# New order of the loads of a fused kernel's front, and 28 identity turns in place of 36

## The chip, the cores and the metric

The kernel runs on one core of a Trainium2 chip. Its engines are TensorE (PE, matrix products), VectorE (DVE), ScalarE (ACT), GpSimd (POOL) and SyncE (SP), which issues DMA transfers. Time is the device time of one execution in microseconds (us); the figure of a kernel is the median of its runs.

## The reference

A small two-way attention between 512 tokens and 32 states per head, for 8 batches and 8 heads, is followed by a gated layer and by a second layer with a tanh. Cut to what is computed:

```python
scores = scale * np.matmul(x, state.transpose(0, 1, 3, 2))      # tokens read the states
a = softmax(scores);  xread = np.matmul(a, state)
scores2 = scale * np.matmul(state, x.transpose(0, 1, 3, 2))     # states read the tokens
a2 = softmax(scores2); sread = np.matmul(a2, x)
x = rows of np.concatenate([xread, sread], axis=2)              # 8 * 544 rows of 512
h = (x @ w1) * (x @ w2) @ w3                                    # w1, w2: 512 x 1024, w3: 1024 x 1024
x = h @ w_out                                                   # 1024 x 512
h = x @ w_in;  return (h - np.tanh(h)) @ w_out2                 # 512 x 2048, 2048 x 512
```

All data are float32. A product is made of three passes over two parts of each operand, a high part (fp32r, written by ScalarE) and a low part (the rest, written by VectorE).

## The kernel before, in words

The stages run one after the other on every engine: the front (`stage_front`), the states' rows (`stage_ys`), the first layer (`stage_moe1`) and the second (`stage_moe2`). Only the front is touched, some 80 us at the start.

The front does three things beside each other. It multiplies w3 by w_out once and for all, in 8 rounds of 4 pieces: round r takes a block of 512 KB of w3 (`load_w3`, L390), split by ScalarE into w3T_hi (L440, L446) and by VectorE into w3T_lo (L563, L568), times the 8 parts k of w_out (`load_wo`, L378; wos_hi L450, wos_lo L573), of which a piece takes two; the matmuls are at L724, and the last of a round raises `prod_done`. It does the states' attention for 8 batches e: `scores` (L682, from xT, the columns of x, 1024 KB a batch, and raising `scored`) into the PSUM room px, ScalarE's copy (L473) and exp (`exp_a2`, L481), PE's turn of it (L690), `sread` (L702, from xs, the rows of x, 1024 KB a batch, raising `sread_done`) and a turn of its result (`sread_turn`, L710), from which ScalarE and VectorE make srs_hi (L500) and srs_lo (L603). And it loads w1 and w2 in 8 parts of 512 KB (`load_w`, L385: four quarters of the rows, w1 and w2 in turn) into a room of their own, w_raw, with no wait ahead. ScalarE's `split_w(0)` (L469) waits for all 8, and VectorE's follows it (L581); these are needed first by `s1` (L752), at the front's end.

PE's order is written out by hand: `warm()` (L670) turns the identity WARM times into px, with no use of the result; then pieces 0 to 4, scores(0), pieces 5 to 7, scores(1), a2_turn(0), and for each further batch e the pieces up to `PIECES_AT[e]`, sread(e - 1), scores(e + 1), sread_turn(e - 2) and a2_turn(e). `scores(e)` also waits until the exp of batch e - 1 has emptied px (L677). At the end come piece 31, sread_turn(6), sread(7), the first value products (L112) and s1.

The orders of ScalarE and VectorE are written out too. ScalarE's, around the first batches, is: empty_prod(0), copy_st(0), split_w3(2), exp_a2(0), empty_prod(1), copy_st(1), turn_a2(0), exp_a2(1), split_w3(3). After the last batch's exp it is split_w(0), split_w(1), copy_sr(6), split_sr(5) and so on, and VectorE's is the same with L603 for split_sr.

SP issues nearly all loads, in its own order, on one queue. Three kinds wait first, because their two buffers are used in turn: xT of batch e for `scored` of batch e - 2, xs of batch e for `sread_done` of batch e - 2, and w3 of round r for `prod_done` of round r - 2. A wait holds up all that stands behind it in SP's order. xT and xs of batches 0 and 1 wait for nothing. ScalarE issues the first w_out load and the first two loads of the states.

Of the kernel before, what the change touches and what calls it, by code (L numbers as in the profile page):

```python
# [51 lines left out]
def after(eng, sem, count):  # L52

    if not (isinstance(count, int) and count <= 0):
        eng.wait_ge(sem, count)
# [14 lines left out]

PASSES = ((0, 0), (0, 1), (1, 0))
LAST = len(PASSES) - 1
WARM = 36
WRING = 3


# [219 lines left out]
def stage_front(nc, sem, room_a, room_b, room_c, room_o, small, w_at, x_rows, x_cols, state_cols, w1, w2, w3_cols, wo, aT, w34_at, w34,  # L296
# [71 lines left out]
    def load_xT(eng, e):  # L368

        after(eng, scored, e - 1)  # L370
        eng.dma_start(xTb[e % 2][:, :, :], x_cols[e]).then_inc(xT_in[e % 2], 16)

    def load_xs(eng, e):

        after(eng, sread_done, e - 1)
        eng.dma_start(xsb[e % 2][:, :, :], x_rows[e]).then_inc(xs_in[e % 2], 16)

    def load_wo(eng, n):  # L378
        ks = slice(WO_LOADS[n][0], WO_LOADS[n][-1] + 1)
        eng.dma_start(wor[:, ks, :], wo.rearrange("(k p) c -> p k c", p=P)[:, ks, :]).then_inc(wo_in[n], 16)  # L380

    def load_sT(eng, n):
        eng.dma_start(sT[:, STATES[n], :, :], state_cols[:, STATES[n], :, :]).then_inc(sT_in[n], 16)

    def load_w(eng, n):  # L385

        q, ab = n // 2, n % 2
        eng.dma_start(w_raw[:, q, ab, :], (w1, w2)[ab][q * P:(q + 1) * P, :]).then_inc(w_in[ab], 16)

    def load_w3(eng, r):  # L390

        after(eng, prod_done, r - 1)
        eng.dma_start(w3r[r % 2][:, :, :], w3_cols[r]).then_inc(w3_in[r % 2], 16)

    def sync(sp):
        def load_first(n):
            sp.dma_start(w3r[0][:, FIRST[n], :], w3_cols[0, :, FIRST[n], :]).then_inc(first_in[n], 16)

        for n in range(2):
            load_first(n)  # L400
        for n in range(1, len(WO_LOADS)):
            load_wo(sp, n)
        load_w3(sp, 1)
        load_xT(sp, 0)
        load_w3(sp, 2)
        load_xT(sp, 1)
        load_xs(sp, 0)
        load_sT(sp, 2)
        load_xT(sp, 2)
        load_w3(sp, 3)  # L410
        load_xs(sp, 1)
        load_xT(sp, 3)
        load_w3(sp, 4)
        load_w(sp, 0)
        for e in range(2, 5):
            load_xs(sp, e)
            load_xT(sp, e + 2)
            load_w(sp, e - 1)
            if e < 4:
                load_w3(sp, e + 3)  # L420
        load_xs(sp, 5)
        load_xT(sp, 7)
        load_w3(sp, 7)
        for n in (4, 5):
            load_w(sp, n)
        load_xs(sp, 6)
        for n in (6, 7):
            load_w(sp, n)
        load_xs(sp, 7)

    def gpsimd(pool):
        pool.memset(ident[:, :], 0.0).then_inc(ident_zeroed, 1)  # L432
# [232 lines left out]
    def tensor(pe):  # L665
        def warm():

            pe.wait_ge(ident_ready, 1)
            for n in range(WARM):
                pe.transpose(px[:, 0:P], ident[:, :], ident[:, :])  # L670
# [109 lines left out]
        for f in range(NF1):  # L780
            s1(f)

    return {"sync": sync, "gpsimd": gpsimd, "scalar": scalar, "vector": vector, "tensor": tensor,
            "signals": (pst, s1_done, s1_pm, s1_lo)}

# [695 lines left out]
```

## Time and profile before

| | us |
|---|---|
| median of 3 runs | 1248.16 |
| lowest and highest | 1247.09, 1248.64 |
| the profiled execution, its time | 1246.85 |
| its span, first to last instruction | 1245.1 |
| PE busy | 1237.0 |
| VectorE busy, ScalarE busy | 800.1, 548.5 |
| mean granted clock of PE | 1.000 |

The page gives the busy time of each engine as a share of the span. The share says which engine could be the bound; where it is not quite 100%, the list of waits says who made it stand. Times of the timeline count from the span's start. In it, a number in brackets is the idle time of the engine ahead of the instruction, and after the arrow stands what ended it. A matmul's end is modelled, and the next one begins before it, so the distance of two starts is the pace. "To landing" of a load is counted from the start of its issue on SP to the moment when its semaphore is raised.

### The profile page before, as it was taken

The page shows a single profiled execution, that of the slowest core. Times are in us where ns is not written, and L with a number is a line of the kernel's source. Part 1 is how long each engine was busy: PE and PEld are TensorE (multiplying, and loading weights), DVE is VectorE, ACT ScalarE, POOL GpSimd, SP SyncE. Part 2 cuts the span into 40 slices and gives each one's busy share as a digit, 9 for nine tenths or more (in the row PEclk, how much of TensorE's full clock was granted, in tenths as well). Part 3 has the DMA queues.
Part 4 walks back from the last instruction along what each step waited for, and adds up shares of the span by engine and source line. Part 5 has one row for each costly group of instructions (what it writes and reads, how often), then busy time and mean ns, then how long its engine had stood idle before and what let it go on. Part 6 is the DMA issues. An engine that isn't in the chain of part 4 may idle for free.

```text
span 1245.1 us, 17116 instructions
## 1 busy us (share of the span) xinstructions
PE 1237.0 (99%) x6636; PEld 1004.5 (81%) x6636; DVE 800.1 (64%) x1295; ACT 548.5 (44%) x1028; POOL 1.3 (0%) x7
## 2 busy tenths in 40 slices
PE   9999999999999999999999999999999999999998
PEld 7779777777777778888888888888888888888887
DVE  4656556555555445878676676676676776766776
ACT  6663434333333334555444444444444444444444
POOL 0000000000000000000000000000000000000000
PEclk9999999999999999999999999999999999999999
DMA  9941000000000111311101001001001001010000
GB/s 354 372 172 52 35 34 1 34 35 1 34 35 1 68 71 49 93 60 34 51 18 40 12 18 52 1 18 51 0 17 51 8 8 51 17 42 0 9 34 18
DMA packets 17630, 63.76 MB, mean 51 GB/s; under 512 B 1968, under 2 KB 3376, under 8 KB 12960
## 3 DMA queue, kind: packets, MB, share of 16 engines
q1 hardware_dynamic: 16832, 62.00, 13.6%
q8 instruction: 40, 0.66, 0.2%
q10 hardware_dynamic: 704, 0.85, 0.2%
q14 instruction: 22, 0.18, 0.0%
q0 software_dynamic: 32, 0.07, 0.0%
HBM read 45.09 MB, written 17.83 MB: 51 GB/s over the span
## 4 chain that ended last, share of the span: by engine, by line
issue 100%; POOLq 0%; POOL 0%
POOLq L261 0%; POOL ident L434 0%; POOL ident L432 0%; POOLq L434 0%; POOLq L1469 0%
## 5 line engine op out<-in xcount | busy, mean ns | idle before, releaser
L1256 ACT ACTIVATE hq<-bank 128x512 f32<-128x512 f32 (+1 forms) x144 | 82.8, 575 | 393.8 <-PE bank L1382 393.8
L1327 DVE TENSOR_TENSOR hw<-hw,hq 128x512 f32<-128x512 f32 (+1 forms) x144 | 95.5, 663 | 193.5 <-ACT hw L1267 193.4
L1382 PE MATMUL bank<-ysp_hi,wi_hi 128*128 128x512 f32 (+1 forms) x576 | 217.4, 377 | 0.0
L1382 PE MATMUL bank<-ysp_lo,wi_hi 128*128 128x512 f32 (+1 forms) x576 | 217.2, 377 | 0.0
L1382 PE MATMUL bank<-ysp_hi,wi_lo 128*128 128x512 f32 (+1 forms) x576 | 217.2, 377 | 0.0
L1409 PE MATMUL wide<-wz_hi,gsp_hi 128*128 128x512 f32 x544 | 212.3, 390 | 0.3 <-DVE gsp_lo L1317 0.3
L1409 PE MATMUL wide<-wz_lo,gsp_hi 128*128 128x512 f32 x544 | 211.8, 389 | 0.0
L1409 PE MATMUL wide<-wz_hi,gsp_lo 128*128 128x512 f32 x544 | 211.7, 389 | 0.0
L1382 PEld LDWEIGHTS bank<-ysp_hi,wi_hi 128*128 128x128 f32 x576 | 108.2, 188 | 21.3 <-DVE gb L1346 0.9
L1382 PEld LDWEIGHTS bank<-ysp_lo,wi_hi 128*128 128x128 f32 x576 | 108.3, 188 | 20.6
L1382 PEld LDWEIGHTS bank<-ysp_hi,wi_lo 128*128 128x128 f32 x576 | 108.3, 188 | 19.9
L1409 PEld LDWEIGHTS wide<-wz_hi,gsp_hi 128*128 128x128 f32 x544 | 102.2, 188 | 22.2 <-DVE gsp_lo L1317 1.4
L1409 PEld LDWEIGHTS wide<-wz_hi,gsp_lo 128*128 128x128 f32 x544 | 102.1, 188 | 21.4
L1409 PEld LDWEIGHTS wide<-wz_lo,gsp_hi 128*128 128x128 f32 x544 | 102.1, 188 | 20.4
L1317 DVE TENSOR_TENSOR gsp_lo<-gb,gsp_hi 128x512 fp32r<-128x512 f32 (+1 forms) x144 | 95.5, 663 | 13.4 <-ACT gsp_hi L1249 0.5
L1071 PE MATMUL wide<-psp_hi,w_hi 128*128 128x512 f32 x256 | 101.5, 396 | 0.1
L1344 DVE COPY_PREDICATED gb<-far,wide 128x512 f32<-128x512 uint8 (+1 forms) x144 | 100.9, 701 | 0.2
L1071 PE MATMUL wide<-psp_lo,w_hi 128*128 128x512 f32 x256 | 99.8, 390 | 0.0
L1071 PE MATMUL wide<-psp_hi,w_lo 128*128 128x512 f32 x256 | 99.6, 389 | 0.0
L1346 DVE TENSOR_TENSOR gb<-bank,gb 128x512 f32<-128x512 f32 (+1 forms) x144 | 95.3, 662 | 5.0
L1334 DVE SCALAR_TENSOR_TENSOR gb<-hw,bank 128x512 f32<-128x512 f32 (+1 forms) x144 | 93.8, 651 | 0.1
L1249 ACT ACTIVATE gsp_hi<-gb 128x512 fp32r<-128x512 f32 (+1 forms) x144 | 86.2, 599 | 3.5 <-DVE gb L1346 3.3
(122 smaller groups left out, 1740.7 us busy)
## 6 DMA issues: line engine op xcount, KB each, us to landing
xT<-in_x_cols SPq DMA_DIRECT2D x8, 1024.0 KB, 10.2
xs<-in_x_rows SPq DMA_DIRECT2D x8, 1024.0 KB, 9.6
y_dram<-ysb SPq DMA_DIRECT2D x8, 1024.0 KB, 3.9
out<-ysb SPq DMA_DIRECT2D x8, 1024.0 KB, 4.6
yr<-y_dram SPq DMA_DIRECT2D x28, 256.0 KB, 4.0
w_raw<-in_moe_w SPq DMA_DIRECT2D x8, 512.0 KB, 11.2
wi_raw<-in_moe_w_in SPq DMA_DIRECT2D x4, 1024.0 KB, 6.5
raw<-in_moe_w_out SPq DMA_DIRECT2D x16, 256.0 KB, 2.6
```

The lines of the kernel that those rows point to most:

```text
L1071: mm = pe.matmul(py[c], w34[s][:, f, c * P:(c + 1) * P], psp[t][:, f % 2, :], start=f + m == 0, stop=f == NF1 - 1 and m == LAST)
L1249: act.activation(gsp[0][:, slot, 0:w], gb[:, slot % 2, 0:w], ACT.Copy).then_inc(g_hi, 1)
L1256: act.activation(hq[:, f % 2, 0:w], ph[f % 2][:, 0:w], ACT.Square).then_inc(sq_done, 1)
L1317: dve.tensor_tensor(gsp[1][:, slot, 0:w], g, plain(gsp[0][:, slot, 0:w]), ALU.subtract).then_inc(g_lo, 1)
L1327: dve.tensor_tensor(u, u, q, ALU.mult).then_inc(w2_done, 1)
L1334: dve.scalar_tensor_tensor(g, u, 1.0, h, ALU.add, ALU.mult).then_inc(near_done, 1)
L1344: dve.copy_predicated(g, far[:, f % 2, 0:w], pq[f % 2][:, 0:w]).then_inc(sel_done, 1)
L1346: dve.tensor_tensor(g, h, g, ALU.subtract).then_inc(g_done, 1)
L1382: mm = pe.matmul(ph[f % 2][:, 0:w], wi[s][c][:, f * P:(f + 1) * P], ysp[k][u][c][:, 0:w], start=c + m == 0, stop=c == KC - 1 and m == LAST)
L1409: mm = pe.matmul(po[j], gsp[s][:, f % 4, j * P:(j + 1) * P], wz[u][:, f, :], start=f + m == 0, stop=f == NF2 - 1 and m == LAST)
```

## The change

SP's order of the front's loads is rewritten. xT of batch 1 goes ahead of w3 of round 2. The halves of w1 and w2 come earlier: two ahead of w3 of round 4, two ahead of round 5, one each ahead of rounds 6 and 7 and the last two behind xT of batch 7. xs of batch 5 goes ahead of w3 of round 7 and xT of batch 7 behind it, and xs of batch 6 behind the last halves. The waits that each load carries stay as they are, and so do the number of loads and their sizes. WARM falls from 36 to 28.

```diff
-WARM = 36
+WARM = 28
@@ sync of stage_front
         load_w3(sp, 1)
-        load_xT(sp, 0)
+        for e in range(2):
+            load_xT(sp, e)
         load_w3(sp, 2)
-        load_xT(sp, 1)
         load_xs(sp, 0)
         load_sT(sp, 2)
         load_xT(sp, 2)
         load_w3(sp, 3)
         load_xs(sp, 1)
         load_xT(sp, 3)
+        for n in (0, 1):
+            load_w(sp, n)
         load_w3(sp, 4)
-        load_w(sp, 0)
-        for e in range(2, 5):
-            load_xs(sp, e)
-            load_xT(sp, e + 2)
-            load_w(sp, e - 1)
-            if e < 4:
-                load_w3(sp, e + 3)
+        load_xs(sp, 2)
+        load_xT(sp, 4)
+        for n in (2, 3):
+            load_w(sp, n)
+        load_w3(sp, 5)
+        load_xs(sp, 3)
+        load_xT(sp, 5)
+        load_w(sp, 4)
+        load_w3(sp, 6)
+        load_xs(sp, 4)
+        load_xT(sp, 6)
+        load_w(sp, 5)
         load_xs(sp, 5)
+        load_w3(sp, 7)
         load_xT(sp, 7)
-        load_w3(sp, 7)
-        for n in (4, 5):
-            load_w(sp, n)
-        load_xs(sp, 6)
         for n in (6, 7):
             load_w(sp, n)
-        load_xs(sp, 7)
+        for e in (6, 7):
+            load_xs(sp, e)
```

## Rows read from the trace of the kernel before

**Rows 1.** The page, busy time, share and instructions of each engine.

```profile
PE 1237.0 (99%) x6636; PEld 1004.5 (81%) x6636; DVE 800.1 (64%) x1295; ACT 548.5 (44%) x1028; POOL 1.3 (0%) x7
```

**Rows 2.** Waits of PE, whole run: waited for, us in total, times, longest.

```profile
PE wide L670 <- POOL ident L434: 1.5, 1, 1.5
PE wide L710 <- DVE srs_lo L603: 1.4, 1, 1.4
PE bank L724 <- DVE w3T_lo L568: 0.4, 1, 0.4
...
PE wide L682 <- DMA xT<-in_x_cols: 0.3, 1, 0.3
```

**Rows 3.** Timeline of SP: start us, us, engine, line, operation.

```profile
4.82 0.44 SPq L371 DMA_DIRECT2D xT<-in_x_cols  x1
13.73 0.33 SPq L393 DMA_DIRECT2D w3r<-in_w_cols  x1
...
20.80 0.43 SPq L376 DMA_DIRECT2D xs<-in_x_rows  x1
21.59 0.33 SPq L371 DMA_DIRECT2D xT<-in_x_cols  x1
```

**Rows 4.** DMA issues, the same four in turn: KB each, us to landing.

```profile
xT<-in_x_cols SPq DMA_DIRECT2D x1, 1024.0 KB, 9.5
...
w3r<-in_w_cols SPq DMA_DIRECT2D x1, 512.0 KB, 3.9
...
xs<-in_x_rows SPq DMA_DIRECT2D x1, 1024.0 KB, 10.0
...
xT<-in_x_cols SPq DMA_DIRECT2D x1, 1024.0 KB, 11.7
```

**Rows 5.** Windows of 1 us: busy per engine, PE clock, DMA share, GB/s.

```profile
14.00:15.00 1.00, 1.00 (x7) 0.57 (x5) 0.63 (x1) 0.34 (x1) 0.00 (x0) 1.00 0.29 49
...
40.00:41.00 1.00, 1.00 (x6) 0.81 (x6) 0.97 (x4) 0.65 (x2) 0.00 (x0) 1.00 0.37 115
```

**Rows 6.** Timeline of ScalarE: w_out, w3 of round 2, exp_a2(0), split_w(0).

```profile
7.85 3.33 ACT L450 ACTIVATE wos_hi<-wor 128x512 fp32r<-128x512 f32 x6 [0.90 <-DMA wor<-in_moe_w_out]
...
17.66 1.06 ACT L446 ACTIVATE w3T_hi<-w3r 128x1024 fp32r<-128x1024 f32 x1 [0.45 <-DMA w3r<-in_w_cols]
...
19.95 0.20 ACT L481 ACTIVATION_READ_ACCUMULATOR a<-wide,tbias 128x1 f32 x1
...
74.85 2.01 ACT L469 ACTIVATE w_hi<-w_raw 128x1024 fp32r<-128x1024 f32 x2 [1.60 <-DMA w_raw<-in_moe_w]
```

**Rows 7.** Timeline of VectorE: the later six wos_lo, and srs_lo before 78.9.

```profile
8.52 3.70 DVE L573 TENSOR_TENSOR wos_lo<-wor,wos_hi 128x512 fp32r<-128x512 f32 x6 [0.58 <-ACT wos_hi L450]
...
78.50 0.27 DVE L603 TENSOR_TENSOR srs_lo<-wide,srs_hi 128x128 fp32r<-128x128 f32 x1
```

**Rows 8.** Timeline of PE: first product, scores(0), scores(1), and from 78.9.

```profile
7.49 0.48 PE L724 MATMUL bank<-wos_hi,w3T_hi 128*128 128x512 f32 x1
...
9.35 0.47 PE L724 MATMUL bank<-wos_hi,w3T_hi 128*128 128x512 f32 x1 [0.23 <-DVE wos_lo L573]
...
14.67 0.39 PE L724 MATMUL bank<-wos_hi,w3T_lo 128*128 128x512 f32 x1
14.99 1.09 PE L682 MATMUL wide<-xT,sT 64*32 64x512 f32 x16
...
20.01 0.39 PE L724 MATMUL bank<-wos_hi,w3T_lo 128*128 128x512 f32 x1
20.41 1.09 PE L682 MATMUL wide<-xT,sT 64*32 64x512 f32 x16
...
78.91 0.30 PE L710 MATMUL wide<-ident,sr 128*128 128x128 f32 x1 [1.39 <-DVE srs_lo L603]
79.14 1.10 PE L702 MATMUL wide<-xs,a2T 128*32 128x64 f32 x64
```

**Rows 9.** Timeline of PE, the identity turns: to 5.3 us, and after 5.7 us.

```profile
1.53 4.10 PE L670 MATMUL wide<-ident 128*128 128x128 f32 x18 [1.53 <-POOL ident L434]
...
5.43 2.19 PE L670 MATMUL wide<-ident 128*128 128x128 f32 x17
```

## The prediction

> **What bounds the kernel now.** I read the shares by engine first [rows 1]: TensorE (PE) is busy in 1237.0 of a 1245.1 us span, so the change can win only idle time of PE, and only in the front, since no other line of code is touched. Then the waits of PE over the whole run [rows 2]. They are few: 1.5 us for the identity at the very start, 1.4 us at L710 for VectorE's srs_lo, 0.4 at L724 for w3T_lo, 0.3 at L682 for an xT load, 0.2 at L724 for wos_lo. The rest of the 8.1 us lies after the front or behind PE's last instruction. Everything past about 82 us goes PE's pace, so what the front gives or costs reaches the end of the run unchanged.
>
> Third, what stands behind these waits. They are transfers. The one queue of SyncE (SP) lands its loads in the order of issue, and with a backlog the landings stand 2.5 us apart per 1024 KB: the load issued at 20.80 lands at 30.8, the next, issued at 21.59, at 33.3 [rows 3, 4]. Half a megabyte takes 1.25. But the DMA engines are not always fed: their share drops to 0.29 between 14 and 15 us, because SP, having issued xT of batch 0 at 4.82, waits until 13.73 for prod_done before w3 of round 2, and xT of batch 1 stands behind that wait [rows 3, 5]. There is another hole at 40 us (0.37), and a slack stretch from 49 to 53 us. What is lost there is missing at the end: the last w lands at 74.7; ScalarE, free since 73.25, has sat 1.60 us for it and starts split_w(0) at 74.85; and the chain split_w, split_w, VectorE's L603 (78.50 to 78.77) lets PE go on at 78.91 [rows 6 to 8].
>
> **Part 1, the order of loads.** I redo the queue with those paces: a load lands 2.5 us per MB after the one ahead of it, but not sooner than a load issued to an empty queue, which is 3.9 us for 512 KB (w3 of round 2 [rows 4]). The sT load in small packets and the xT behind it keep the 4.4 us that they take together now. A time "before" is the start of the issue plus its time to landing; of some 30 such pairs four stand in [rows 3, 4].
>
> Issued early, xT of batch 0 lands at 14.3 as before (4.82 + 9.5) and xT of batch 1, now right behind it, at 16.8 in place of 20.1. Then w3 round 2 at 18.05 (before 17.6), xs0 20.6, xT2 24.9 (before 27.0), w3 round 3 26.2, xT3 31.2, w of w1 and w2 33.7, w3 round 4 34.9 (before 34.5), xT4 39.9, two more halves of w1 and w2 42.4. These halves are what sits in the queue when SP gets past prod_done for round 5 at 39.8: it lands at 43.9 (before 44.1) and the hole at 40 us is gone. xs3 46.5, xT5 49, w 50.3. At 48.4 w3 round 6 meets a queue as shallow as before, so I take most of that loss over: 52.7 (before 53.0), xs4 between 54.8 (at pace) and 57.1 (as before), taken 56.3 since the nearest rows are the old ones. From there a backlog holds: xT6 58.8 (before 59.7), xs5 62.5, w3 round 7 63.8 (before 67.2), xT7 66.3 (before 66.0), the last w 68.8 (before 74.7), xs6 71.3 (before 72.2), xs7 73.9 (before 77.2).
>
> Now PE's stalls. (a) 0.3 us (0.27 in PE's timeline) for xT6 at 59.7 goes [rows 2]: it lands 0.9 us earlier. (b) 0.4 us (0.38) at 69.6 for w3T_lo of round 7 goes: the load is 3.4 us earlier, and ScalarE, which now sits 1.7 us for it, splits it that much sooner. (c) 1.39 us at 78.9: with the last w in by 68.8, ScalarE starts split_w(0) when it is free, at 73.25 and not 74.85 [rows 6]. From that start to the end of L603 it takes 78.77 - 74.85 = 3.9 us, so L603 ends at 77.2. PE's idle time of 1.39 before 78.91 starts at 77.5 [rows 8], so PE could go on there. It fits with some 0.2 us to spare: PE's order, not VectorE, is late next. Sum: 2.04 us won.
>
> (d) A new wait is made. w3 round 2 now stands behind a megabyte more: 18.05 in place of 17.6. ScalarE waits for it already (L446 at 17.66, idle 0.45 before), and behind L446 in its order stands exp_a2(0), whose last piece ends at 20.15 [rows 6]. scores(1) on PE reuses px and waits for that exp (L677); it starts at 20.41, 0.40 after the last matmul's start, where scores(0) took 0.32 (14.67 to 14.99), so no slack is left there [rows 8]. I charge the full 0.45 us. Bounds: 0, if the fuller queue moves w3 sooner than the sum says, and 0.55. Other loads that land later than now (w3 round 4 by 0.4, xT7 by 0.3 at most 1.1) have over 1 us and, xT7, 0.7 us before PE needs them at 67.01, and 0.2 to 0.4 us at worst would show. The SP issues themselves are as many as before, 0.33 to 0.44 us each, and no wait is added; xT7 and xs5 change sides of the wait for prod_done of round 7, but the queue has over 5 us of backlog then.
>
> Part 1: -2.04 + 0.45 = -1.6 us.
>
> **Part 2, 28 turns for 36.** The first 18 start 0.217 us apart (1.53 to 5.22), the later ones 0.12 (the 17 from 5.43 end at 7.62, the last of 0.27 us) [rows 9]. This is TensorE's clock going from 1.2 to 2.4 GHz at some 5.5 us, after 4 us of work, though the granted clock reads 1.00 throughout. Eight late turns are 8 x 0.12 = 0.96 us, so the product could start at 6.53 and not 7.49. It can: the first wos_lo is there at 6.4, on a row of VectorE's that is not shown. But after two k (1.4 us) PE needs the third wos_lo, made from a wor load for which ScalarE waits until 7.85, the first of the six that VectorE writes from 8.52 on, 0.62 us each; PE starts on it at 9.35 now and will start on it at 9.35 then [rows 6 to 8]. So in this execution the 0.96 us only turn the gap of 0.23 into one of about 1.2 us: worth 0.
>
> In other executions it may be worth something. If the clock rises later than at 5.5 us, each turn costs 0.217: 36 of them at that step end at 9.3, 28 end at 7.6. The product would then reach the third k at up to 10.8 with 36 turns and still about in time with 28. So part 2 is worth 0 to 1.4 us; the only row I have says 0, and the median of before is 1.3 us above the profiled execution, so I take 0.3.
> The Trainium skill (TensorE: Matmul & The Clock Gate, Part 1: The HAM clock gate) says that the half rate is the default, that sustained activity releases it, and that the point where it is released differs from run to run. The trace agrees on the two rates; no run here shows yet whether the point moves. By that page fewer turns with a longer gap behind them speak against this change; the third rival below is what that would do here.
>
> **The sum.** Against the profiled execution (span 1245.1, time 1246.85): 1246.85 - 1.6 = 1245.3, without part 2. The median of the three runs is 1248.16; with part 2: 1248.16 - 1.6 - 0.3 = 1246.3 us.
>
> **Rivals.**
> 1. The new wait does not come, or part 2 is worth its upper part: -2.04 and -0.3 to -1.0, 1245.4 us. For it: DMA engines that finish early pass on to the next load, and the sum goes by the slowest. Against: ScalarE waits for exactly this load today. 0.22.
> 2. The 1.4 us stall is only renamed: PE waits at L710, or for xs7 at the next step, because the margin at 77.5 is 0.2 us and xs4 to xs6 come late. Then only (a) and (b) count: -0.65 + 0.45 = -0.2, 1247.9 us. Against: ScalarE is idle 1.60 us there, and every input but w is in place. 0.12.
> 3. Slower: the clock falls back in the gap of 1.2 us near 8 to 9.3 us. Price: at the start PE ran 4.0 us at half rate; a second such stretch costs half of it, 2.0 us, and pushes everything behind it, w3 round 2 too. -1.6 + 2.0 = +0.4, 1248.6 us, and more if the low level lasts on; it decides from the moment when two such stretches occur, or one costs over 1.6 us. Against: PE idled 1.39 us at 77.5 and came back at full pace (64 matmuls of L702 in 1.10 us, as everywhere) [rows 8]. 0.06.
> 4. The change does nothing to the time: the holes refill elsewhere (49 us, behind the new w halves) and the last w lands late all the same. 1248.1 us. It would take over 4 us of new loss, and the holes of today together cost 6. 0.04.
>
> **How the numbers follow.** Forecast 0.56, rivals 0.22, 0.12, 0.06, 0.04. 0.2% is 2.5 us, about the least that a measurement can tell from no change. The forecast, 1.9 us, lies inside, and so do rivals 2 and 4; rival 1 (2.8 us) is mostly beyond. With the scatter of the median runs (1247.09 to 1248.64) I give faster 0.24, same 0.73, slower 0.03. The range runs from 1244.9 (rival 1 with most of part 2) to 1248.2 (rival 2 and the scatter).
>
> **What would show it.** In the profile after: no stall at L682 near 59, at L724 near 69 and at L710 near 77; ScalarE's L469 starts right behind the last L481, near 73; DMA share near 1 from 13 to 16 us; the last w in by 69; L446 of round 2 at about 18.1 and scores(1) at about 20.85; L724 starts at 6.5 and has its gap of 1.2 us up to 9.35; weight loads of 0.19 us right after it. Wrong would be: matmuls of L724 over 0.3 us apart after 9.35 (rival 3), scores(1) still at 20.41 (rival 1), or L710 waiting for srs_lo or L702 for xs (rival 2).

## The result, and the profile after

The changed kernel takes 1252.16 us (median of 10 runs, 1250.26 to 1254.21) against 1247.74 for before (10 runs): ratio 1.0036, interval 1.0027 to 1.0046. It is slower by 4.4 us where a gain of 1.9 was forecast. The profiled execution took 1250.26 us, its span is 1248.5, 3.4 more than before's.

The page of the changed kernel, shares and instruction packets, and the same queue's row of before, 40 packets:

```profile
PE 1236.2 (99%) x6628; PEld 1002.8 (80%) x6628; DVE 800.8 (64%) x1295; ACT 548.5 (44%) x1028; POOL 1.3 (0%) x7
...
q8 instruction: 58, 0.95, 0.3%
```

```profile
q8 instruction: 40, 0.66, 0.2%
```

TensorE is busy as long as before [rows 1], so the loss is idle time. PE's waits in the changed kernel, which answer to [rows 2] (its lines are numbered 5 higher: L675 for L670, L729 for L724, L1387 for L1382):

```profile
PE bank L1387 <- issue: 4.2, 2, 2.1
PE wide L675 <- POOL ident L439: 1.5, 1, 1.5
PE bank L729 <- DVE wos_lo L578: 1.5, 2, 1.3
PE wide L687 <- ACT a L486: 0.8, 1, 0.8
```

The three stalls of the front that the change aimed at are gone (L715 for srs_lo, L729 for w3T_lo, L687 for xT). In their place stand a wait at L687 for ScalarE's exp, 0.8 us, and, first in the list, two waits of 2.1 us at L1387, in the second layer, with no releaser at all. Nothing of the diff is there.

The front gained what it should. The next rows are from the timelines: SP, where the states' rows are stored, first in the kernel before and then in the changed one; and of the changed kernel ScalarE's split of w3 round 2 and split_w(0), and PE:

```profile
118.75 0.66 SPq L794 DMA_DIRECT2D y_dram<-ysb  x1
```

```profile
117.18 0.66 SPq L799 DMA_DIRECT2D y_dram<-ysb  x1
```

```profile
18.65 1.06 ACT L451 ACTIVATE w3T_hi<-w3r 128x1024 fp32r<-128x1024 f32 x1 [1.34 <-DMA w3r<-in_w_cols]
...
73.31 2.00 ACT L474 ACTIVATE w_hi<-w_raw 128x1024 fp32r<-128x1024 f32 x2
```

```profile
9.47 0.47 PE L729 MATMUL bank<-wos_hi,w3T_hi 128*128 128x512 f32 x1 [1.32 <-DVE wos_lo L578]
...
21.30 1.09 PE L687 MATMUL wide<-xT,sT 64*32 64x512 f32 x16 [0.80 <-ACT a L486]
...
77.36 0.30 PE L715 MATMUL wide<-ident,sr 128*128 128x128 f32 x1
```

ScalarE splits w at 73.31 with no idle time ahead, where [rows 6] had 74.85; PE is at L715 at 77.36, not 78.91 [rows 8]. At 117 us the changed kernel leads by 118.75 - 117.18 = 1.57 us. By the end it is 3.4 behind: 5.0 us are lost after that, in two places. The first one, PE's timeline:

```profile
839.49 0.49 PE L1387 MATMUL bank<-ysp_hi,wi_hi 128*128 128x512 f32 x1
839.82 0.40 PE L1387 MATMUL bank<-ysp_lo,wi_hi 128*128 128x512 f32 x1
842.28 0.50 PE L1387 MATMUL bank<-ysp_hi,wi_lo 128*128 128x512 f32 x1 [2.07 <-issue]
```

The second is its twin at 1018.78. L1387 there is the first step of `tile(2 * i, 0)`, inside the only loop that TensorE runs as a loop, `with pe.Fori(1, PAIRS)` in `stage_moe2`: three rounds, so two jumps back. After each jump PE gets two matmuls done and stands; from start to start it is 842.28 - 839.82 = 2.46 us where 0.23 is usual. Around the jump the DMA engines carry nothing but code. The changed kernel between 836 and 846 us; the first line is the DMA engines' share in 40 slices of 0.25 us, and its three digits stand for packets at 836.8, 839.9 and 844.1:

```profile
DMA  0002000000000002000000000000000020000000
DMA packets 3, 0.05 MB, mean 5 GB/s; under 512 B 0, under 2 KB 0, under 8 KB 0
q8 instruction: 3, 0.05, 1.9%
```

In the same ten microseconds of the kernel before no packet moves at all. From 845 to 1200 us the changed kernel fetches 15 such packets, and before none. 0.95 MB in 58 packets is 16 KB each.

The trace also holds TensorE's branch instruction itself (the timeline above leaves such instructions out). At its two jumps back it takes 3.40 and 3.29 us in the changed kernel, begun at 835.81 and 1012.41, and 0.24 and 0.22 us in the kernel before. During the branch PE still works off matmuls that were handed to it earlier, up to the one at 839.24, so that wait does not show. What shows is the next one: the branch ends at 839.2, two matmuls follow, a packet moves at 839.9, and PE goes on at 842.28.

**Theory A, the layout of the code.** A turn is a weight load and a matmul; PE's count falls by 8 of each. So the loop's code lies 16 instructions earlier, and by this theory its start has slipped over the edge of a fetched block. The loop then touches one block more than TensorE keeps, so each jump back has to wait for code. **Rivals.** B: the new order of loads does it, by when the transfers meet the loop. C: fewer turns are bad as such, through the clock at the start, or in proportion to their number.

### The profile page after: what moved, and what is told of

It reads as the page before. It is cut to its first block, busy times and chain, and to the rows that moved or that the text cites. A ratio compares the mean times of both kernels' runs of the same rounds, so it can differ in the third digit from the quotient of the medians.

```text
span 1248.5 us, 17100 instructions
## 1 busy us (share of the span) xinstructions
PE 1236.2 (99%) x6628; PEld 1002.8 (80%) x6628; DVE 800.8 (64%) x1295; ACT 548.5 (44%) x1028; POOL 1.3 (0%) x7
## 4 chain that ended last, share of the span: by engine, by line
issue 100%; POOLq 0%; POOL 0%
POOLq L261 0%; POOL ident L439 0%; POOL ident L437 0%; POOLq L439 0%; POOLq L1474 0%
## 5 line engine op out<-in xcount | busy, mean ns | idle before, releaser
L1387 PE MATMUL bank<-ysp_hi,wi_lo 128*128 128x512 f32 (+1 forms) x576 | 217.5, 378 | 4.2 <-issue 4.2
L1387 PE MATMUL bank<-ysp_hi,wi_hi 128*128 128x512 f32 (+1 forms) x576 | 217.6, 378 | 0.0
L1387 PE MATMUL bank<-ysp_lo,wi_hi 128*128 128x512 f32 (+1 forms) x576 | 217.3, 377 | 0.0
L1387 PEld LDWEIGHTS bank<-ysp_hi,wi_lo 128*128 128x128 f32 x576 | 108.3, 188 | 24.9 <-issue 5.0
L1387 PEld LDWEIGHTS bank<-ysp_hi,wi_hi 128*128 128x128 f32 x576 | 108.2, 188 | 21.7 <-DVE gb L1351 1.0
L1387 PEld LDWEIGHTS bank<-ysp_lo,wi_hi 128*128 128x128 f32 x576 | 108.3, 188 | 20.4
```

Source lines behind the costliest of these rows:

```text
L1387: mm = pe.matmul(ph[f % 2][:, 0:w], wi[s][c][:, f * P:(f + 1) * P], ysp[k][u][c][:, 0:w], start=c + m == 0, stop=c == KC - 1 and m == LAST)
```

## The experiments

All are compared with runs of before on the same chip, in the same job. Medians of before in the three jobs: 1247.47, 1247.29 and 1247.48 us.

**One part at a time.** The first has the order of before and 28 turns.

```diff
-WARM = 36
+WARM = 28
```

> The order of loads of before, and 28 turns in place of 36. Theory A (code layout): 8 turns fewer are 16 instructions fewer on TensorE ahead of the loop of the second layer, and the loop then starts at the end of a fetched block of code; at each of its two jumps back TensorE stands about 2.1 us for code. Expected: two idle times of about 2.1 us at L1382 by no named releaser, about 58 instruction packets in place of 40, span 1245.1 + 5.0 = 1250, median 5 to 6.5 us above before. Theory B (the new order of loads does it, by shifting when transfers meet the loop): no such idle times here, time as before within 1 us. Theory C (the clock falls after the gap near 8 us): the matmuls of L724 behind 9.4 us stand over 0.3 us apart.

Measured 1253.43 us, ratio 1.0052 (1.0038 to 1.0066): the turns alone cost 6 us. Its page has 58 instruction packets, and among its first waits of PE are

```profile
PE bank L1382 <- issue: 4.6, 2, 2.4
...
PE wide L710 <- DVE srs_lo L603: 1.4, 1, 1.4
```

Theory B falls: the order of loads is that of before, and so is the stall at L710. The second takes the new order and puts the turns back.

```diff
-WARM = 28
+WARM = 36
```

> The new order of loads, and 36 turns. Theory A: TensorE's code has the length of before, so 40 instruction packets, no idle time at L1387, and what the order is worth in the front remains: 1.2 to 1.6 us below before (the stalls of 0.3, 0.4 and 1.4 us gone, a new one of 0.8 us at scores(1)). Theory B: 3.4 us or more above before, with the two idle times.

Measured 1245.82 us, ratio 0.9985 (0.9976 to 0.9994), 40 packets, no wait at L1387. The order alone gains 1.65 us between medians, as the prediction's part 1 had it.

**The same 28 turns at the start, with the length of the code restored.** The 8 turns come back where PE stands idle anyway.

```diff
         warm()
-        pieces(0, 5)
+        pieces(0, 1)
+        for n in range(8):
+            pe.transpose(px[:, 0:P], ident[:, :], ident[:, :])
+        pieces(1, 5)
```

> The new order of loads, 28 turns at the start and the other 8 behind the first piece of the product, where TensorE stands idle for 1.3 us. Theory A: the code ahead of the loop is as long as before, so 40 instruction packets, no idle time at L1387, 1.2 to 1.8 us below before. If it were the 28 turns as work ahead of the first product (the clock, theory C) or the order (B): as the changed kernel, 3.4 us or more above before.

Measured 1245.88 us, ratio 0.9989 (0.9980 to 0.9998), 40 packets, no wait at L1387. This is against C in its plain form: TensorE has as few turns before its first product as in the changed kernel, and nothing is lost. But the 8 turns also fill the gap behind the first product, so this run doesn't say what the gap does. The run with no jump, further down, does: it keeps 28 turns and a gap of 1.30 us, and loses nothing.

**Where the edge is.** The new order with 32, 31 and 30 turns, a step of two instructions for each turn.

```diff
-WARM = 28
+WARM = 32
```

> The new order of loads and 32 turns: 8 instructions fewer than before, 8 more than the changed kernel. In the changed kernel TensorE gets through two matmuls (4 instructions) of the repeated loop before it stands. Theory A: with 8 instructions more ahead, the loop's start lies behind the edge of the block, so no idle time at L1387, 40 packets, 1.2 to 1.8 us below before. A cause that grows with the number of turns taken away would give half of the loss: about 1 to 2 us above before.

> The new order and 31 turns, between 30 (stands for code before the first matmul of each repetition) and 32 (does not). One turn is 2 instructions. All or nothing again: 40 packets and about 2 us below before, or 58 packets and about 5 us above. I expect no stall, since with 30 turns not even one matmul came ahead of it.

> The new order and 30 turns: 4 instructions more than the changed kernel, which gets through 4 instructions of matmuls before it stands, and 4 fewer than the 32 turns, which don't stand at all. Theory A: all or nothing. Either 58 packets and two idle times of about 2.1 us (3.5 to 5 us above before), if one instruction or more of the loop lies ahead of the edge, or 40 packets and 1.5 to 2.5 us below before. A loss between these, about 1 us above before, speaks for a cause that grows with the count.

| turns, new order | median, us | ratio, interval | packets of code |
|---|---|---|---|
| 36 | 1245.82 | 0.9985 (0.9976 to 0.9994) | 40 |
| 32 | 1245.04 | 0.9983 (0.9974 to 0.9992) | 40 |
| 31 | 1245.26 | 0.9984 (0.9974 to 0.9993) | 40 |
| 30 | 1252.95 | 1.0049 (1.0037 to 1.0061) | 58 |
| 28 | 1252.16 | 1.0036 (1.0027 to 1.0046) | 58 |

Between 31 and 30 turns, two instructions of the 17,100 that the page counts for all engines, lie 7.7 us (medians of two jobs whose medians of before differ by 0.2; three of the six runs with 30 turns also hold a fall of the clock, see below, and the other three lie 6.2 to 6.8 us above the median with 31). There is nothing in between, so nothing grows with the count. The place of the wait moves with the count too. By the trace a round opens with two register instructions. With 28 turns these and two matmuls with their weight loads, six instructions, come through before PE stands; with 30 turns the two register instructions alone; with 31 PE doesn't stand. So each turn moves the edge by its two instructions, and with 31 it has reached the loop's start. PE's timeline of the kernel with 30 turns, at its second jump back:

```profile
1016.30 0.39 PE L1414 MATMUL wide<-wz_hi,gsp_lo 128*128 128x512 f32 x1
1019.32 0.79 PE L1387 MATMUL bank<-ysp_hi,wi_hi 128*128 128x512 f32 x1 [2.63 <-issue]
1019.91 0.63 PE L1387 MATMUL bank<-ysp_lo,wi_hi 128*128 128x512 f32 x1
1020.34 0.63 PE L1387 MATMUL bank<-ysp_hi,wi_lo 128*128 128x512 f32 x1
...
1025.46 0.41 PE L1414 MATMUL wide<-wz_hi,gsp_lo 128*128 128x512 f32 x1
```

Here is a second loss, which the profile of the changed kernel doesn't show. After 2.6 us of idle time the matmuls stand 0.43 us apart, not 0.23, until 1025.5. The windows say why (length, PE busy, granted clock, DMA share, GB/s):

```profile
1010.00:1016.00 6.00, 6.00 (x28) 1.00 0.01 3
1019.30:1025.50 6.20, 6.18 (x15) 0.50 0.01 3
1026.00:1032.00 6.00, 6.00 (x28) 1.00 0.00 0
```

TensorE is granted 1.2 GHz from 1018.7, inside the idle time, to 1025.5, 6.8 us in all and 6.2 of them with matmuls, which cost twice their time: about 3 us more. After the first jump of the same execution, 2.45 us idle, the clock stayed. The time from branch to branch gives the full price. It is 174.1 us in the kernel before, 176.6 and 176.5 in the changed one, 176.8 twice in the one with 28 turns alone, and 176.9 and, with the clock's fall, 179.9 here. So the wait for code costs 2.4 to 2.8 us each time, and the fall 3.0 more. It shows in the runs of the changed kernel: those with a mean granted clock of 0.999 took 1250.3 to 1252.6 us, the three with 0.997 took 1253.2 to 1254.2. That does not explain why its median, a run with 0.999, lies 1.9 us above its profiled execution; this stays open. Nor does the fall belong to the wait for code alone: of the 89 runs of before beside these experiments four have a clock of 0.998 and took 1249.2 to 1250.7 us, and what they idled for wasn't profiled.

**No jump.** The changed kernel, 28 turns, with TensorE's three rounds written out.

```diff
-        with pe.Fori(1, PAIRS) as i:
+        for i in range(1, PAIRS):
             tile(2 * i, 0)
             tile(2 * i + 1, 1)
```

> The changed kernel with the repeated part of TensorE's second layer written out three times, so TensorE never jumps back there; all else, 28 turns and the new order, as changed. Theory A (a jump back to code that is no longer held): no idle time at L1387 for code, instruction packets all along (over 58), time 1.5 to 2.5 us below before, as the order with 36 or 32 turns gave. If the loss came of the position of the code as such and not of the jump, or from fetching more code: idle times remain, 3 us or more above before.

Measured 1244.76 us, ratio 0.9983 (0.9974 to 0.9992), no wait at L1387. The packets are 52, not over 58: that number was wrong. Written out, two rounds more cost 12 packets over the 40 of a held loop; the loop that isn't held fetched 18 more, 9 after each jump. The same 52 say that queue q8 carries TensorE's code, since nothing else was changed. In this run straight code came in time, with no idle time at L1387; it is the jump back to a block no longer held that costs. With this, theory A stands on four legs: the turns alone make the loss, padding in another place takes it away, it has an edge of two instructions, and it goes with the jump.

**The number of turns for itself.**

```diff
-WARM = 36
+WARM = 32
```

> The order of before and 32 turns: the number of turns alone, on the good side of the edge. The prediction's term for fewer turns: 0 in an execution whose clock rises early, some 0.2 to 0.5 us below before in the median, since four turns fewer matter only where the clock rises late. If the turns matter for themselves: 0.5 us of gain in every execution, or a loss. 40 instruction packets, no idle time for code.

Measured 1247.37 us, ratio 1.0002 (0.9993 to 1.0011): no gain is seen. The interval, from -0.9 to +1.4 us, is too wide to exclude the 0.2 to 0.5 us. In the new order 32 turns came out 0.78 us below 36 in the same job, and those intervals overlap as well (0.9974 to 0.9992 and 0.9976 to 0.9994). So the turns' own worth stays unsettled, and is under 1 us by all medians.

**The new wait at scores(1).** As the new order with 32 turns, but

```diff
-        for e in range(2):
-            load_xT(sp, e)
+        load_xT(sp, 0)
         load_w3(sp, 2)
+        load_xT(sp, 1)
```

> As the new order with 32 turns, but w3 of round 2 goes ahead of xT of batch 1 again. The wait at scores(1) (0.8 to 0.9 us in the profiles of the new order, for ScalarE's exp behind the split of w3) should go, ScalarE's split of w3 should start at about 17.7 in place of 18.6. If the queue then is late nowhere else: 0.8 us below the new order with 32 turns, 3 us below before. Rival: the hole in the transfers from 13 to 15 us is back, everything behind lands 1 to 2 us later, and the gain is eaten by a wait for xT or w3 between 58 and 70 us; then equal to the new order within 0.3 us.

Measured 1244.82 us, ratio 0.9982 (0.9973 to 0.9991), in another job than the order as it is; so both ran again side by side.

> The new order with 32 turns once more, now beside the form with w3 of round 2 first on the same chip. Expected: 2.0 to 2.5 us below before.

> 32 turns and w3 of round 2 ahead of xT of batch 1, beside the new order as it is on the same chip. If the wait at scores(1) costs what its idle time says, 0.4 to 0.8 us below the other; if it is paid back by later waits, within 0.2 us of it.

The order as it is: 1245.17 us, 0.9982 (0.9973 to 0.9991). w3 first: 1244.84 us, 0.9978 (0.9969 to 0.9987). The two rows of PE's timeline, the order as it is and w3 first:

```profile
20.79 1.09 PE L687 MATMUL wide<-xT,sT 64*32 64x512 f32 x16 [0.34 <-ACT a L486]
```

```profile
20.78 1.09 PE L687 MATMUL wide<-xT,sT 64*32 64x512 f32 x16
```

The wait is gone, though in the second execution PE itself came later there. Between medians it is 0.33 us, less than the 0.4 to 0.8 expected, and the intervals overlap, so the size isn't settled. The idle time at scores(1) in the profiles of the new order is 0.15, 0.22, 0.33, 0.34, 0.34, 0.46, 0.80 and 0.94 us: a wait that differs by execution, of which the changed kernel's profile shows a large one.

Last, both gains together, w3 first and no jump:

> 32 turns, the new order with w3 of round 2 ahead of xT of batch 1, and TensorE's repeated part written out. If the steps found so far add up: no idle time for code whatever the length ahead, no wait at scores(1), 2.5 to 3.2 us below before. Rival: the written-out code gains nothing over the loop that is held; equal to the looped form within 0.3 us.

Measured 1245.03 us, ratio 0.9978 (0.9969 to 0.9987): as w3 first with the loop kept. The gains don't add up, which the rival had right: a loop whose code is held has nothing for the written-out one to gain. Any of these forms beats both kernels by its interval; the smallest step tried from the changed kernel is 31 turns.

## Why the prediction was wrong, point by point

**The step that failed** stands in its first paragraph: that the change can win or lose only in the front, "since no other line of code is touched", and that what the front gives "reaches the end of the run unchanged". The first holds for the lines, not for where the code of the later lines lies. Part 2 was put at 0 to 1.4 us of gain; it is a loss of 6.0 us between medians. In the profile of the turns alone the span is 5.5 us longer, and the two rounds after the jumps back, 2.8 us longer each, are all of it. None of the rivals had this. The third, for the slower side, put the clock's fall at 8 us, behind the shortened turns. The gap was there (1.32 us before 9.47) and the clock held: the matmuls after it stand 0.23 apart. It fell elsewhere, after a gap twice as long.

The rows that would have warned were at hand: 40 packets of 16 KB of code, TensorE the engine with by far the most instructions, a loop in it, and no packet while the loop repeats. A change of TensorE's instruction count ahead of that loop was a step to be costed.

The Trainium skill (Runtime: NRT & Kernel Launch, Instruction fetch mechanics) says that code comes in blocks of 256 instructions, 16 KiB, and that a taken branch to a block that isn't held must wait for a fetch. The trace agrees: 16 KB a packet, 12 packets for the 3152 instructions of two rounds written out, and 2.4 to 2.8 us a jump where packets follow it. The same section of the Trainium skill gives TensorE room for 2048 instructions, which is 8 blocks, and says that a branch must stay within a window of two blocks or wait. By two blocks the kernel before would have to fetch at its jumps too, and it doesn't; the measurement decides.

An estimate with the Trainium skill's block of 256: the trace has 1576 instructions of TensorE from branch to branch, 1536 of them matmuls and weight loads, so a round is 6 blocks and 40 instructions. Begun just behind an edge it touches 7 blocks, begun less than 40 instructions ahead of one, 8. Read so, the runs say that 7 are kept and 8 are not. By the same estimate a start 40 or more instructions ahead of the edge, at 11 turns or fewer, would be held again; no run tried that.

**Part 1 was right, by compensating errors.** The sum said -1.6 us. PE's row at L715 moved from 78.91 to 77.36, and the order alone measured -1.65.
- (b) and (c) went as said: no idle time at L729 near 69.6 or at L715 at 77.36, and split_w(0) at 73.31 against the forecast 73.25. The queue was slower than the sum, though: the last w landed at 70.0 and not by 68.8, which still left over 3 us.
- (a) went by luck. The stall at L687 is gone, but xT6, which was to land 0.9 us earlier than before, landed 0.3 later (issued at 50.91, 9.0 us, so at 59.9; before 49.90 and 9.8). It was in time only because (d) had made PE 0.9 us late, so that it came to L687 at 60.29. In the eight profiles of the new order it landed between 58.3 and 59.9.
- The stalls were worth more than their idle time. From the row at 21.30 (0.89 later than before) to that at 77.36 (1.55 earlier) PE gained 2.44 us, not 2.04. Counted by starts the three stalls were worth 0.34, 0.62 and 1.46 us, where their idle times are 0.27, 0.38 and 1.39: a modelled end reaches past the point where the next matmul could have begun, here by 0.06 to 0.24 us.
- (d), the new wait, came, by the chain that was named, and was mis-sized: 0.80 us in this profile against 0.45, bound 0.55. The split of w3 round 2 started at 18.65, not 18.1, because its load landed at 18.6 (issued 13.83, 4.8 us): the megabyte ahead, due at 16.8, came at 16.9, and the half megabyte behind it took 1.7 us where the steady pace gives 1.25. In other profiles it is 0.15 to 0.94.

**Part 2, the turns for themselves.** In this execution, 0, as said: 28 turns end at 6.34, the product starts at 6.54 (forecast 6.53), and the third k at 9.47 (before 9.35). The further 0.3 us for executions whose clock rises late are not shown: 32 turns measured 1.0002, with an interval that is wider than the term. The premise, that the rise moves, holds. 36 turns took 6.20 us in the profile of before and 6.91 in that of the new order with 36. There the product started 0.71 us later than before, and the third k 0.32 later, at 9.67: the gap ahead of it took in the rest.

**The chances.** Slower by over 0.2% had 0.03. All cases came from the front; for the place where the time was lost there was none.

## What to carry to other kernels

Before adding or removing instructions ahead of a loop of TensorE (no other engine's loop was tried here), look where the packets of code fall: if they stop while the loop repeats, its code is held, and a few instructions ahead of it can push it over an edge, at 2.4 to 2.8 us a jump here and now and then 3 more for the clock. An idle time with the releaser "issue" right behind a jump, with a packet of code beside it, is the mark. When a small change moves time far from its own lines, put the length of the code back with work in a gap, or write the loop out, before you look for a cause in the data.

## What the runs showed of the hardware that I had not expected

- A loop of TensorE of 1576 instructions a round repeats with no fetch of code at all (no packet from 845 to 1200 us before), or fetches 15 in that stretch, by its place alone.
- The wait for code at a jump back is 2.1 to 2.6 us of idle time in the three profiles that have it. The branch itself takes 3.3 to 3.5 us there and 0.2 where the loop is held, and PE's work in hand hides that part.
- In one of the six waits of these profiles, the longest with 2.63 us, the granted clock fell to 0.50 (1.2 GHz) for 6.8 us; in the others, 2.07 to 2.45 us, it stayed at 1.00, and so it did at idle times of 1.3 to 1.5 us in the front.
